# Attention lead of a fused fp32 kernel: first unit's keys in 128-token chunks, coarse softmax steps moved between engines

## The reference

```
q_d, k_d, v_d = mean of 4 tokens each                 # 144 coarse tokens per head
out_d  = softmax(q_d k_d^T / 8) v_d, repeated 4 times # coarse attention
out_l  = softmax(q k^T / 8 where |i-j| < 4) v         # local attention
x      = out_d + out_l                                # [B, S, 512]
x      = x + relu(layernorm(x) @ w_ch1) @ w_ch2       # 512 -> 2048 -> 512
xk, xr = mixtures of x and the token before
out    = sigmoid(xr @ w_r) * (relu(xk @ w_k)**2 @ w_v)
```

## Time and profile before

| | us |
|---|---|
| median of 3 runs (lowest, highest) | 763.57 (763.51, 763.83) |
| the profiled execution, its own time | 763.69 |
| its span in the trace | 761.1 |
| PE busy in the span | 751.0 |
| the lead, up to the first matmul of `up_b` | 34.09 |
| DVE, ACT, POOL busy in the span | 432.3, 272.7, 231.1 |

### The profile page before, as it was taken

How to read it: one execution, slowest core, us unless ns; L and a number is a source line. 1 busy time by engine, 2 the same in 40 slices (tenths; PEclk the granted TensorE clock), 3 DMA queues, 4 the chain that set the end, 5 groups by cost and what they waited for, 6 DMA issues and landing times.

```text
span 761.1 us, 15855 instructions
## 1 busy us (share of the span) xinstructions
PE 751.0 (99%) x6457; PEld 692.5 (91%) x6457; DVE 432.3 (57%) x805; ACT 272.7 (36%) x620; POOL 231.1 (30%) x268
## 2 busy tenths in 40 slices
PE   7999999999999999999999999999999999999998
PEld 6799999999999999999999999998888888888886
DVE  5686863544644344654354332657786776766655
ACT  3765432322323233233233231556344434333322
POOL 5668752233343233344224222004111111111101
PEclk9999999999999999999999999999999999999999
DMA  9793541230540121441011005612002010010010
GB/s 202 200 306 70 106 91 21 35 77 16 96 100 9 23 63 40 74 91 41 13 26 40 15 2 174 197 56 88 1 14 97 1 59 25 1 55 1 1 55 28
DMA packets 116543, 49.67 MB, mean 65 GB/s; under 512 B 95084, under 2 KB 105592, under 8 KB 116472
## 3 DMA queue, kind: packets, MB, share of 16 engines
q1 hardware_dynamic: 116472, 48.68, 25.0%
HBM read 39.20 MB, written 9.45 MB: 64 GB/s over the span
## 4 chain that ended last, share of the span: by engine, by line
PE 97%; DVE 1%; POOL 1%; ACT 0%; issue 0%; DVEq 0%; POOLq 0%; ACTq 0%
PE psH L1099 28%; PE psY L1116 27%; PE psH L1150 13%; PE psY L1171 13%; PE psA L1132 6%; PE psA L1027 2%; PE psA L996 2%; PE psA L928 1%; PE psA L972 1%; PE psA L1007 1%; PE psA L941 1%; PE psA L912 0%; PE psA L1032 0%; DVE xc_lo L1630 0%; PE psY L947 0%
## 5 line engine op out<-in xcount | busy, mean ns | idle before, releaser
L1099 PE MATMUL psH<-xc_hi,w_hi 128*128 128x288 f32 x512 | 155.4, 303 | 1.0 <-DVE xc_lo L1630 1.0
L1116 PE MATMUL psY<-h_hi,w_hi 128*128 128x288 f32 x512 | 152.6, 298 | 0.0
L1099 PE MATMUL psH<-xc_hi,w_lo 128*128 128x288 f32 x512 | 151.0, 295 | 0.0
L1099 PE MATMUL psH<-xc_lo,w_hi 128*128 128x288 f32 x512 | 151.0, 295 | 0.0
L1116 PE MATMUL psY<-h_lo,w_hi 128*128 128x288 f32 x512 | 150.7, 294 | 0.0
L1116 PE MATMUL psY<-h_hi,w_lo 128*128 128x288 f32 x512 | 150.7, 294 | 0.0
L1771 DVE SCALAR_TENSOR_TENSOR h_lo<-psH,h_hi 128x288 fp32r<-128x288 f32 x128 | 58.2, 455 | 161.3 <-ACT h_hi L1467 160.8
L1467 ACT ACTIVATE h_hi<-psH 128x288 fp32r<-128x288 f32 x128 | 52.5, 410 | 242.6 <-PE psH L1099 242.0
L897 POOL TENSOR_TENSOR relu_k<-relu_k 128x512 f32<-128x512 f32 (+1 forms) x39 | 38.7, 992 | 243.7 <-ACT relu_k L1422 243.7
L1099 PEld LDWEIGHTS psH<-xc_hi,w_hi 128*128 128x128 f32 x512 | 96.1, 188 | 4.1 <-issue 2.7
L1116 PEld LDWEIGHTS psY<-h_hi,w_hi 128*128 128x128 f32 x512 | 96.0, 188 | 1.4 <-issue 1.1
(11 more groups left out here) (191 smaller groups left out, 1348.6 us busy)
## 6 DMA issues: line engine op xcount, KB each, us to landing
w_raw<-in_moe_w_ch_dram SPq DMA_DIRECT2D x8, 1024.0 KB, 8.0
v_win<-in_v_dram SPq DMA_DIRECT2D x84, 56.0 KB
x_scratch<-x SPq DMA_DIRECT2D x8, 576.0 KB, 4.3
out_dram<-gate SPq DMA_DIRECT2D x17, 256.0 KB, 2.2
raw<-in_q_dram SPq DMA_DIRECT2D x112, 36.0 KB, 2.1
raw<-in_k_dram SPq DMA_DIRECT2D x96, 36.0 KB, 1.9
v_raw<-in_v_dram SPq DMA_DIRECT2D x12, 288.0 KB
x_sh<-x_scratch SPq DMA_DIRECT2D x3, 1026.0 KB, 5.7
```

What stands on the lines that cost most here:

```text
L1099: ins = mm(psH[:, m % 2, 0:N], ws[a][:, kt, f * P:(f + 1) * P], xx[bb][:, kt], start=(kt == 0 and i == 0), stop=(kt == KT - 1 and i == 2))
L1116: ins = mm(psY[:, d, 0:N], ws[a][:, f, d * P:(d + 1) * P], hs[bb][:, m % 2], start=(f == 0 and i == 0), stop=(f == NF1 - 1 and i == 2))
```

## The change

It rewrites the lead only.

- The keys of unit 0 come in chunks of 128 tokens: two, two, and a last one of 64 (the new `turn_tokens`), with five DMAs in place of six. `scores(0, 1)` now needs only the first key step, `scores(0, 2)` the second.
- ScalarE copies the third key step before the first exponential; VectorE sums it before `sum_of_p(0, 0)`.
- TensorE makes the coarse scores before `scores(0, 2)`; `add_values` is split in two halves, one before `scores(0, 2)`, the other behind the transpose of the first coarse probabilities. `turn_p(0, 0)` comes behind both. `values_d` is one step for both parts.
- VectorE takes the coarse tops before `mask(0, 1)`, and a new `norm_d_first` on VectorE takes the place of GpSimd's `norm_d` in the lead.
- GpSimd's first two `lo_w1_first` wait until VectorE has summed the last window (`last_summed`).
- The `keep_on` matmuls are laid anew, all 256 columns wide. The banks of the steps are dealt anew.

Its core (the lists FIRST and the order on PE are shown as rows further down):

```diff
-             ("S", 0, 1, 2), ("S", 0, 2, 3), ("Sd", 0, 0, 0), ("Sd", 0, 1, 1), ("PT", 0, 0, 2), ("PdT", 0, 0, 0), ("PdT", 0, 1, 1),
+             ("S", 0, 1, 2), ("Sd", 0, 0, 0), ("Sd", 0, 1, 1), ("S", 0, 2, 2), ("PdT", 0, 0, 0), ("PT", 0, 0, 3), ("PdT", 0, 1, 1),
...
     def parts_of(kind, u, n):
-        return TOGETHER.get((kind, n), (n,)) if u else (n,)
+        return TOGETHER.get((kind, n), (n,)) if u or kind == "OD" else (n,)
...
-    TURN = {"Tk": [(0, 1), (2, 3), (4, 5)], "Tq": [(0,), (1, 2)]}
+    TURN = {"Tk": [(0, 1), (2, 3), (4,)], "Tq": [(0,), (1, 2)]}
+
+    def turn_tokens(what, n):
+
+        size = P if what == "Tk" else W
+        t0 = TURN[what][n][0] * size
+        return t0, min(size, (S if what == "Tk" else N) - t0), len(TURN[what][n])
...
-        k_first = sb(L, "k_first", [P, WIN_B, E])
+        k_first = sb(L, "k_first", [P, -(-S // P), E])
...
             sub(0, 2)
-            norm_d(0, 0)
-            norm_d(0, 1)
             norm(0, 1)
             norm(0, 2)
             x_sum(0, 0)
             x_sum(0, 1)
+
+            pool.wait_ge(last_summed, 1)
             lo_w1_first(0)
...
-            def add_values():
-                for half in range(2):
-                    g = 2 * half + 1
-                    wait_v_sum_in(pe, 0, g)
-                    for t in range(FACTOR):
...
+            def add_values(half):
+                g = 2 * half + 1
+                wait_v_sum_in(pe, 0, g)
+
+                wait_step_out(pe, place_of["Tk", 0, 1])
+                for t in range(FACTOR):
...
-                if u == 0 and n == 1:
+                if u == 0:
                     pe.wait_ge(vd_first, 1)
...
-                    pe.wait_ge(turn_out, max(turn_of["Tq", 0, min(n, 1)], turn_of["Tk", 0, min(n, 1)]) + 1)
+                    pe.wait_ge(turn_out, max(turn_of["Tq", 0, min(n, 1)], turn_of["Tk", 0, n // 2]) + 1)
...
             def added_o():
-                act.wait_ge(v_added, 1)
+                act.wait_ge(v_added, 2)
...
+            turn_o("Tk", 2)
             exp_p(0, 0)
-            turn_o("Tk", 2)
             exp_d(0, 0)
             exp_d(0, 1)
+            pdt_o(0, 0)
             exp_p(0, 1)
+            added_o()
             exp_p(0, 2)
             pt_o(0, 0)
-            added_o()
-            pdt_o(0, 0)
             pdt_o(0, 1)
...
+            def norm_d_first(n):
+                p = coarse(prob_slot("Sd", 0, n), 0, n).rearrange("p a j c -> p (a j) c")
+                dve.wait_ge(d_inv, n + 1)
+                nc.vector.tensor_tensor(p, p, inv_d[0:GU, n].unsqueeze(2).to_broadcast([GU, 4, SD]), ALU.mult).then_inc(d_normed, 1)
...
             sum_of_p(0, 0)
-            sum_first("Tk", 2)
-            mask(0, 1)
             top_of_d(0, 0)
             top_of_d(0, 1)
+            mask(0, 1)
+            sum_of_d(0, 0)
+            norm_d_first(0)
             mask(0, 2)
-            sum_of_d(0, 0)
             sum_of_d(0, 1)
+            norm_d_first(1)
```

More of the change, by code:

```diff
@@ L504, in turn_source @@
         def turn_source(what, n, x):
-            return (k_first if what == "Tk" else q_first)[0:W, TURN[what][n][x]]
+            return (k_first if what == "Tk" else q_first)[0:turn_tokens(what, n)[1], TURN[what][n][x]]
         def local(u, n):
@@ L908, in turn @@
                 wait_bank_out(pe, i)
+                size = turn_tokens(what, n)[1]
                 for x in range(len(TURN[what][n])):
@@ L1451, in _ @@
             pt_o(0, 2)
-            od_o(0, 1)
             hi_weight("w1", 0, 0)
```

59 lines of the change are left out of this document (30 added, 29 removed), and 4 rows, old and new, of the table FIRST.

## The result

| | before | changed |
|---|---|---|
| median, us (13 executions each) | 763.71 | 770.18 |
| lowest, highest | 763.20, 765.82 | 765.87, 775.30 |
| the profiled execution, its own time | 763.69 | 766.53 |
| its span | 761.1 | 764.0 |
| first `up_b` matmul in it | 34.09 | 36.98 |

The ratio is 1.0084, with a 95% interval of 1.0055 to 1.0114: slower, as forecast, but by 6.5 us and not by 3.4. The median lies above the stated range (765.0 to 768.3); the profiled execution lies in it. So the one profile doesn't explain the median. The single times tell more: five executions lie at 765.9 to 767.2, three at 770.1 to 770.3, five at 773.6 to 775.3. Of the kernel before, 110 executions beside the experiments have one above 768 (769.1).

A forecast was written before the change was run, and what follows sets the result against it. TensorE's chain bounds the kernel, so the start of the first up_b matmul decides: last AV 3.35 us later, up_b at 37.4 instead of 34.09. Median 763.57 + 3.4 = 767.0 us; range 765.0 to 768.3.

The forecast's parts named there:

- Leg 1: Launch to coarse scores: these start at 15.5 instead of 15.03, 0.5 us later.
- Leg 2: Coarse scores to first coarse transpose (PdT0): two GpSimd operations hold norm_d_first(0), so PdT0 starts at 22.55, 1.0 us later.
- rival B: One hold only: norm_d_first(0) goes between sub(0, 1) and v_sum(0, 2), first coarse transpose at 21.4, 765.9 us; chance 0.25.
- the second hold: Second norm_d_first may be held by sub(0, 2) to about 25.3, second coarse transpose (PdT1) at 25.8, covered by value sums.
- Leg 3: First coarse transpose (PdT0) to last AV: 8.95 us instead of 6.65, 2.3 us longer.
- the 2.2 us of moved work: TensorE work (1.73 + 0.48), done before while waiting for the coarse probabilities, now stands behind them.
- The tail: Last AV to first up_b matmul: 5.92 us that the change hardly touches.
- D: TensorE's clock is up from the start of the lead: 1.9 us gained, 763.5 with no hold, not slower; chance 0.05.
- E: More waits: tail's low part of x held by GpSimd, 768.2, or clock rises only behind first value sum; chance 0.07.

The follow-up runs named there:

- e13: e12's order on the changed kernel without any of its added unread matmuls: median 765.9 us, 4 of 9 executions above 768.
- e12: Changed kernel, scores(0, 2), mask(0, 1) earlier, turn_p(0, 0), add_values(1) ahead of turn_d(0, 0), unread matmuls added: 764.56 us, ratio 1.0007.
- e2: Changed kernel with unread matmuls added before the first coarse transpose and before up_b: median 766.28 us, 3 of 12 above 768.
- e3: Changed kernel with first local transpose and second half of the value sums ahead of the first coarse transpose again: median 771.1 us, 4 of 6 above 768.
- e1: The changed kernel once more, unedited: median 768.31 us, ratio 1.0070.
- e4: Changed kernel with the coarse multiplication on GpSimd again, behind sub(0, 2): median 777.56 us, 5 of 5 above 775.
- e9: Kernel before with only the coarse scores moved ahead of scores(0, 2) on TensorE: median 765.0 us, 3 of 12 above 768.
- e10: Changed kernel with scores(0, 2) ahead of the coarse scores again and mask(0, 1) ahead of the coarse tops: median 769.2 us, 6 of 8 above 768.
- e14: e10 with four unread matmuls in the gap before the first coarse transpose: median 766.4 us, 3 of 8 above 768.
- e15: Kernel before with second half of the value sums and first local transpose behind the first coarse transpose: median 773.1 us, 6 of 6 above 768.
- e5: Changed kernel with unread matmuls in every TensorE gap of over 0.15 us in the lead: median 766.59 us, 1 of 12 above 768.
- e8: Kernel before with five unread matmuls from 1.5 us on, before the first keys come: 764.06 us, ratio 0.9999.

## Why the prediction was wrong

**Leg 1 held.** Start 5.53 (5.5), copy 1.01 (1.0), coarse scores 15.50 (15.5).

**Leg 2: rival B was right, not the forecast.** `norm_d_first(0)` took 1.32 us and PdT0 started at 21.50, not 22.55; B had 21.4. The rule of the Trainium skill, SBUF — State Buffer, "Who interferes with whom", by which one operation holds the other up for its whole length, agrees with the first multiplication here. The second was passed over by two GpSimd operations end to end, 0.62 us behind the second of them: the letter of the rule doesn't say who goes next, and the two multiplications show both answers. I had called the second hold covered by the value sums. It was not quite: PdT1 waited the last 0.19 us for it.

**Leg 3: the sum was nearly right, its reason was not.** From PdT0 to the last AV it took 9.51 us, where I had 8.95. But I called the 2.2 us of moved work the heart. With that work moved back, PdT1 has nothing to wait for on TensorE and waits for VectorE instead: 0.70 us in e13, 1.10 in e12. How little the order is worth shows between e2 and e13, in whose profiles the coarse scores start alike (15.43 and 15.51, both in 0.71): PdT1 starts at 24.35 with the work behind PdT0 and at 23.91 with it in front, 0.44 us apart, and e13 has one hold fewer on VectorE besides. And e3's two lowest executions, at 766.5 and 766.7, aren't below the changed kernel's. So at an even clock VectorE's queue holds the changed lead as much as TensorE's sum does: mask and top of window 2 stand between the two coarse multiplications, and both of those are held. PdT1 comes 2.32 us later than before (24.94 against 22.62); behind it to `up_b` it is another 0.57. These two are the whole 2.89. The tail took 5.97, against 5.92.

**In sum, at the same clock,** the first `up_b` matmul was 36.98 (forecast 37.4) and the span 764.0 (764.5). That it came so near is in part luck: leg 2 was 1.05 us shorter than forecast and leg 3 0.56 longer. The lowest executions differ by 2.6 us (765.8 and 763.2), where I had 3.4 for all.

**The step that failed is the clock, in rivals D and E.** I asked only whether the level could rise sooner, and, in E, whether it rises behind the first value sum, with 0.07 for that and another wait together, and set the second aside: "while PdT0 is late that is covered". I had myself forecast TensorE idle from 19.9 on, and didn't ask whether the level could fall there. The sum has no term for it, and that term is 4 to 9 us in 14 of 25 executions. By their mean clock it rose late in 6 of them and fell in 8. At the lower level a matmul of the lead takes 1.6 to 1.9 times as long (rows of e3). The rise at about 17 was one execution's reading and no constant: in the five profiles with the same order on TensorE up to the first value sum it came near 17.5 (changed, e1), near 13 (e2, e4) and beyond 41 (e3). The Trainium skill, TensorE: Matmul & The Clock Gate, section "Part 1: The HAM clock gate (the "warmup" mystery)", says that the same kernel shows different numbers of slow matmuls from run to run, and that this penalty is under 1% of a typical kernel. The runs agree with the first. They go beyond the second: the longest executions with a mean clock of 1.00, at 774.0 to 775.5 against 766, are 1.0 to 1.2% longer.

**What is shown, and what isn't.** Shown: coarse scores ahead of `scores(0, 2)` bring executions of the first kind, on the kernel before alone (3 of 12 in e9, none in 110 without), and with `scores(0, 2)` in front again there are none (0 of 36 in e10, e12, e13 and e14, 6 of 25 in the changed kernel). The gap of 0.83 us that e9 has there isn't needed: e3's profile is of this kind with 0.26. The half of the value sums behind the coarse transpose, with TensorE waiting ahead of it, brings executions of the second kind, on the kernel before alone (e15, with the longer wait said there). With both stretches closed neither occurs (e12).

Not shown: what in a stretch decides. Gap lengths don't sort the kernels (1.02 us in e10 with falls, 1.10 in e12 without), and neither does being busy (e3 was busy for 12 us at the lower level). The time of the first rise is a rival that no run separates: in seven profiles the level was up before 16 us, and in five of these it fell again (e4, e5, e13, e14 and e15, not e2 and e12); in the ten others it fell again in one (e10). e12 also adds unread matmuls of full width, and e13 (4 of 9 above 768, e12 0 of 11) shows that these belong to the cure; which of them is needed, and whether they work by closing gaps or by the early rise, wasn't tried.

## What to carry to other kernels

A lead that runs alone is tuned to TensorE's clock too: moving work off a stretch where TensorE was busy can cost more through the clock than the order can give (4 to 9 us here, in 14 of 25 executions), and one profile doesn't show it. Look at the single times for groups before explaining a median, and read the level from the lengths of like matmuls, not from the granted clock alone. When a step goes from one engine to another, write down the new engine's whole queue up to the second such step, not only up to the first.

## What the runs showed of the hardware that I had not expected

- TensorE's clock stayed at the lower level for 15 us of unbroken work, most of it small matmuls: from 25 to 40 us in e4, and for 12 us in e3, from 15.5 to beyond 27.
- The granted clock reads 1.00 before the first rise, although like matmuls take nearly twice as long (3.69 and 1.96 us, e3 and the changed kernel).
- 2.5 us of matmuls ahead of the first keys moved the rise by nothing (e8).
- A VectorE operation with two inputs in SBUF, 0.76 us long with GpSimd idle (e10), that waits for GpSimd's operation can go next (1.32 us, and GpSimd's next one is stretched from 1.27 to 1.78) or be passed over once more (1.95 us), in one execution.
- With the same order on TensorE, the clock's first rise came near 13, near 17.5 or beyond 41 us in different executions.
